# Making the mask and rise tables on the chip, and splitting the first w2 on two engines

## The chip, the cores and the metric

The program runs on one core of a Trainium2 chip. The metric is the time of one execution on the device, in microseconds, lower being better. TensorE (PE in the rows), VectorE (DVE), ScalarE (ACT), GpSimd (POOL) and SyncE (SP) each run their own instruction stream in order and wait for each other through semaphores. DMAs are issued from SyncE's and ScalarE's streams (SPq and ACTq) and are carried by the core's 16 DMA engines.

## The reference

Three stages follow each other. Stage 1 is causal attention with decay (retention): each head has its own gamma, and batch is 2, heads 8, sequence 768, head dimension 64. Stages 2 and 3 are mixtures of experts (8 and 4 experts) over the 1536 x 512 result; stage 2's gates are balanced by eight rounds of row and column normalization.

```python
gamma = 1.0 - 2.0 ** (-5.0 - np.arange(H))
for t in range(S):
    state = gamma[None, :, None, None] * state + einsum('bhd,bhe->bhde', k[:, :, t], v[:, :, t])
    y[:, :, t] = scale * einsum('bhd,bhde->bhe', q[:, :, t], state)
...
for e in range(E):
    h = np.maximum(x @ w1[e], 0.0)
    ye = h @ w2[e]
    out += P[:, e:e + 1] * ye
```

## The kernel before, in words

Stage 1 works in 12 steps, one per chunk of 128 positions and batch (step s is chunk s // 2, batch s % 2). In a step TensorE forms the scores of all 8 heads (`score`, L991), multiplies the raised queries with the running state (L1019, from chunk 1 on), adds this chunk's keys and values to the state in PSUM (L1031, the "kv" part), and multiplies the masked scores with the values (L1037, the "y" part; the last three stand in `attend`, L1004). The scores of step s + 1 are formed before step s is attended to. VectorE multiplies the scores by a table `mask`, which holds gamma to the power of the lag, the scale, and zero above the diagonal (`mask_scores`, L624). GpSimd multiplies the keys by `kdecay` (L349) and the queries by a table `rise` (L362). ScalarE makes the next chunk's `rise` from the one before by a factor `step` (L444).

The tables come from memory. `mask` (512 KB) and `rise` (256 KB) stand in SyncE's queue among the loads of queries, keys and values: the mask behind the keys of step 0, the rise table ahead of step 2. `kdecay`, `step` and the gate weights `wg_raw` are small loads from ScalarE's queue. There are buffers for four steps, so the loads of step 4 wait until step 0 is done (`y_done`), and so on. TensorE first runs 8 matmuls on a zeroed tile (`warm`, L1042), whose results nobody reads, and 3 more after each of the first two `score` calls.

A semaphore wait heads nearly each of these operations; what matters here is that scores need `qk_in` (queries and keys of the step landed) and, from step 2, the masking of two steps before.

From the last steps on, stage 2 begins. Every f32 matrix is split in a high part and a remainder (`x_hi`, `x_lo`; `low`, L666), and a product is three fast matmuls. The first matrix product of an expert's half (`up`, L1094) uses seven sub-products in the manner of Strassen, each in two halves; TensorE's seventh waits for `summed`, which VectorE's `hidden_sum` (L804) raises. `down` (L1134) multiplies with w2, whose parts VectorE makes in `split_w2` (L714). VectorE's own order at this place is written out by hand: the last pieces of x and w1, then all of the first w2 (which has landed in a buffer of its own, `w2_first`), then `hidden(0, 0)`. The rest of the program, about 1480 us, repeats units of `up` and `down`.

Of the kernel before, what the change touches and what calls it, by code (L numbers as in the profile page):

```python
# [14 lines left out]
P = 128  # L15
# [18 lines left out]
WARM, WARM_GAP = 8, 3  # L34
# [27 lines left out]
def retention_moe_moe_kernel(nc, q_t, k_t, k, v, moe_w_gate, moe_w1, moe_w2, moe2_probs, moe2_w1, moe2_w2,  # L62
                             c_ident, c_kdecay, c_mask, c_rise, c_step, out):

    ctx = ExitStack()
    with ctx:
# [15 lines left out]
        with ExitStack() as early:  # L82
            mask = sb("mask", [P, 2, DC, P], F32, early)
            rise = [sb(f"rise{r}", [P, DC, P], F32, early) for r in range(2)]
        w2_hi = sb("w2_hi", [P, UC, DM], F32R)
# [13 lines left out]
        kdecay = sb("kdecay", [P, CH - 1, HEADS])  # L99
        step = sb("step", [P, DC])  # L100
# [36 lines left out]
        ps_kv, ps_y = bank[4], bank[5:8]  # L137
        ps_logit = [bank[6], bank[0]]
# [3 lines left out]
        kdecay_in = sem("kdecay_in")  # L142
        wg_in = sem("wg_in")
        mask_in = sem("mask_in")
        rise_in = sem("rise_in")
# [103 lines left out]
        def _(sp):  # L249
# [93 lines left out]
        def _(pool):  # L343
# [9 lines left out]
            def raise_q(s):  # L353

                c, b = s // BATCH, s % BATCH
                pool.wait_ge(qk_in[c % 2][b], 32 * (c // 2) + 32)
                if c == 1:
                    pool.wait_ge(rise_in, 32)
# [32 lines left out]
            pool.wait_ge(kdecay_in, 16)  # L391
# [24 lines left out]
        def _(act):  # L416
            act.dma_start(kdecay[:, :, :], c_kdecay.rearrange("p (c h) -> p c h", c=CH - 1)).then_inc(kdecay_in, 16)
            act.dma_start(step[:, :], c_step).then_inc(rise_in, 16)
            act.dma_start(wg_raw[:, :, :], moe_w_gate.rearrange("p (c e) -> p c e", e=E1)).then_inc(wg_in, 16)
# [33 lines left out]
            def rise_out(c):  # L453

                if c == 2:
                    act.wait_ge(rise_in, 32)
# [44 lines left out]
            gate_weights()  # L501
            for s in range(STEPS):
# [40 lines left out]
            def unit(k, p, x2=None, first=False):  # L543
# [71 lines left out]
        def _(dve):  # L615
# [98 lines left out]
            def split_w2(k, first=False):  # L714
                raw = w2_first if first else w2_raw
                dve.wait_ge(w2_in, 16 * k + 16)
                if not first:

                    dve.wait_ge(down_done, downs_before(k, 0))
# [12 lines left out]
            dve.wait_ge(mask_in, 16)  # L732
            mask_scores(0)
            dve.wait_ge(wg_hi_ready, 1)
            low(wg_parts[:, :, 64 + E1:64 + 2 * E1], wg_raw[:, :, :], wg_parts[:, :, 64:64 + E1])
            low(wg_parts[:, :, P + E1:P + 2 * E1], wg_raw[:, :, :], wg_parts[:, :, P:P + E1]).then_inc(wg_lo_ready, 1)
            for s in range(STEPS):
# [12 lines left out]
                elif b == 1:  # L750
                    if c < CH - 1:
                        x_low0(c)
                    if c > 0:
                        sums_low(c - 1)
            x_low0(CH - 1)
# [57 lines left out]
            def hidden(k, p, x2=None):  # L813
# [62 lines left out]
            split_w2(0, first=True)  # L876
            hidden(0, 0)
# [100 lines left out]
        def _(pe):  # L978
# [63 lines left out]
            def warm(n):  # L1042

                for i in range(n):
                    nc.tensor.matmul(bank[7][:, 0:P], state[1][:, 0, :], state[1][:, 0, :], start=True, stop=True)
# [165 lines left out]
def _constants():  # L1211
# [6 lines left out]
    lag = pos[None, :] - pos[:, None]  # L1218
    mask = np.where(lag >= 0, gamma[:, None, None] ** np.maximum(lag, 0.0), 0.0) / np.sqrt(HD)
    mask = mask.reshape(DC, 2, P, P).transpose(2, 1, 0, 3)  # L1220
    rise = gamma[:, None] ** (P + 1.0 + pos - SEQ // 2)[None, :] / np.sqrt(HD)
    rise = np.repeat(rise.reshape(DC, 2, 1, P), HD, axis=2).reshape(DC, P, P).transpose(1, 0, 2)
    step = np.repeat((gamma ** float(P)).reshape(DC, 2, 1), HD, axis=2).reshape(DC, P).transpose(1, 0)
    return {
        "c_ident": np.eye(P), "c_kdecay": kdecay.reshape(P, (CH - 1) * HEADS), "c_mask": mask.reshape(P, HEADS * P),
        "c_rise": rise.reshape(P, DC * P), "c_step": step,
# [37 lines left out]
```

## Time and profile before

| | us |
|---|---|
| median of 3 runs | 1552.88 |
| lowest and highest | 1552.87, 1552.95 |
| profiled execution | 1552.96 |
| its span, first to last instruction | 1551.2 |
| TensorE busy | 1543.7 |
| VectorE busy | 880.9 |
| ScalarE busy | 445.2 |
| GpSimd busy | 53.8 |

The span is from the first to the last instruction; the execution's own time has some 1.8 us more around it. TensorE is busy for nearly the whole span, so the reader should look at the few places where it isn't, and at what it is busy with before them: a warming matmul counts as busy too.

### The profile page before, as it was taken

The numbers are of one execution on the slowest core, as the hardware profiler recorded it, in microseconds if no ns is written. First come the engines' busy times: TensorE is split into PE (matmuls) and PEld (weight loads), VectorE is DVE, ScalarE is ACT, GpSimd is POOL, SyncE is SP. The second block draws the span as 40 slices with busy tenths as digits, with TensorE's granted clock in tenths as the row PEclk, the third lists the DMA queues.
The fourth block names the chain that finished last, engine by engine and source line by source line (L and its number), as shares of the span: only waits on it lengthen the run. The fifth ranks groups of instructions, "written<-read, shape, count | busy, mean of one in ns | idle before, by whom it ended". The sixth has DMA issues, their size and how long they took to land.

```text
span 1551.2 us, 21289 instructions
## 1 busy us (share of the span) xinstructions
PE 1543.7 (100%) x8238; PEld 1401.2 (90%) x8238; DVE 880.9 (57%) x1439; ACT 445.2 (29%) x860; POOL 53.8 (3%) x45
## 2 busy tenths in 40 slices
PE   8999999999999999999999999999999999999999
PEld 7989988998899889988998899889998999899988
DVE  6756855546546555465465555567555556555553
ACT  5422331322223213222232132243332223213321
POOL 5300000000000000000000000012000000000000
PEclk9999999999999999999999999999999999999999
DMA  9201101001011010010110100101101001011011
GB/s 341 78 1 55 55 2 55 28 28 55 1 54 54 0 54 27 27 54 2 52 54 0 54 29 26 55 0 55 51 4 55 28 28 55 0 54 54 1 41 68
DMA packets 34891, 67.28 MB, mean 43 GB/s; under 512 B 2320, under 2 KB 2704, under 8 KB 34832
## 3 DMA queue, kind: packets, MB, share of 16 engines
q1 hardware_dynamic: 34400, 66.42, 12.5%
q8 instruction: 41, 0.67, 0.2%
q14 instruction: 18, 0.15, 0.0%
q10 hardware_dynamic: 432, 0.04, 0.0%
HBM read 63.31 MB, written 3.15 MB: 43 GB/s over the span
## 4 chain that ended last, share of the span: by engine, by line
PE 98%; DVE 1%; DMA 0%; SPq 0%; ACT 0%; issue 0%; DVEq 0%
PE bank L1148 17%; PE bank L1149 17%; PE bank L1147 17%; PE bank L1126 15%; PE bank L1130 15%; PE bank L1128 15%; PE bank L999 1%; PE bank L1019 1%; PE bank L1037 1%; PE bank L1031 0%; DVE w_lo L667 0%; DMA qt_in<-in_q_t 0%; PE bank L1090 0%; DVE w_hi L722 0%; DVE x_sum L636 0%; PE bank L1071 0%
## 5 line engine op out<-in xcount | busy, mean ns | idle before, releaser
L1126 PE MATMUL bank<-x_hi,w_hi 128*128 128x384 f32 x1344 | 449.9, 335 | 0.4 <-DVE ups L805 0.4
L1130 PE MATMUL bank<-x_hi,w_lo 128*128 128x384 f32 x1344 | 449.5, 334 | 0.0
L1128 PE MATMUL bank<-x_lo,w_hi 128*128 128x384 f32 x1344 | 449.2, 334 | 0.0
L1149 PE MATMUL bank<-w_hi,h_lo 128*128 128x512 f32 x1148 | 447.6, 390 | 0.0
L1148 PE MATMUL bank<-w_lo,h_hi 128*128 128x512 f32 x1148 | 447.4, 390 | 0.0
L1147 PE MATMUL bank<-w_hi,h_hi 128*128 128x512 f32 x1148 | 446.9, 389 | 0.0
L852 DVE SCALAR_TENSOR_TENSOR acc<-bank,gate,acc 128x512 f32<-128x512 f32 x251 | 188.5, 751 | 372.7 <-PE bank L1149 372.7
L538 ACT COPY ups<-bank 128x384 f32<-128x384 f32 x288 | 138.0, 479 | 902.8 <-PE bank L1130 902.7
L805 DVE TENSOR_TENSOR ups<-bank,ups 128x384 f32<-128x384 f32 x288 | 155.4, 555 | 190.1 <-ACT ups L538 168.4
L1149 PEld LDWEIGHTS bank<-w_hi,h_lo 128*128 128x128 f32 x1148 | 215.4, 188 | 44.9
L1148 PEld LDWEIGHTS bank<-w_lo,h_hi 128*128 128x128 f32 x1148 | 215.4, 188 | 43.8
L1147 PEld LDWEIGHTS bank<-w_hi,h_hi 128*128 128x128 f32 x1148 | 215.5, 188 | 43.6
L1126 PEld LDWEIGHTS bank<-x_hi,w_hi 128*128 128x128 f32 x1344 | 252.3, 188 | 2.9 <-issue 1.1
L1128 PEld LDWEIGHTS bank<-x_lo,w_hi 128*128 128x128 f32 x1344 | 252.3, 188 | 1.8
L1130 PEld LDWEIGHTS bank<-x_hi,w_lo 128*128 128x128 f32 x1344 | 252.2, 188 | 0.0
L541 ACT ACTIVATE h_hi<-ups 128x384 fp32r<-128x384 f32 x288 | 148.3, 526 | 135.7 <-DVE ups L805 135.7
L810 DVE SCALAR_TENSOR_TENSOR h_lo<-ups,h_hi 128x384 fp32r<-128x384 f32 x288 | 156.3, 557 | 12.3
L667 DVE TENSOR_TENSOR w_lo<-w_raw,w_hi 128x1024 fp32r<-128x1024 f32 (+1 forms) x95 | 112.7, 1207 | 0.0
L810 DVE SCALAR_TENSOR_TENSOR h_lo<-bank,h_hi 128x384 fp32r<-128x384 f32 x96 | 53.5, 558 | 2.2
L541 ACT ACTIVATE h_hi<-bank 128x384 fp32r<-128x384 f32 x96 | 47.3, 493 | 12.5
L367 POOL TENSOR_TENSOR x_lo<-x_sum,x_hi 128x1024 fp32r<-128x1024 f32 x7 | 17.9, 2559 | 894.3 <-ACT x_hi L442 894.3
L667 DVE TENSOR_TENSOR w_lo<-w_sum,w_hi 128x1024 fp32r<-128x1024 f32 (+1 forms) x48 | 46.4, 966 | 0.0
(96 smaller groups left out, 508.4 us busy)
## 6 DMA issues: line engine op xcount, KB each, us to landing
w_raw<-in_moe_w SPq DMA_DIRECT2D x46, 1024.0 KB, 5.0
kt_in<-in_k_t SPq DMA_DIRECT2D x12, 256.0 KB, 3.9
qt_in<-in_q_t SPq DMA_DIRECT2D x12, 256.0 KB, 5.2
v_in<-in_v SPq DMA_DIRECT2D x12, 256.0 KB, 5.6
k_in<-in_k SPq DMA_DIRECT2D x10, 256.0 KB, 5.4
out<-acc SPq DMA_DIRECT2D x2, 768.0 KB, 3.5
out<-acc SPq DMA_DIRECT2D x5, 256.0 KB, 2.0
w_raw<-in_moe_w SPq DMA_DIRECT2D x4, 256.0 KB, 5.6
```

Of the source, the lines that this page charges most:

```text
L538: nc.scalar.copy(ups[:, half, slot, :], up_psum(ON_X, half)).then_inc(copied, 1)
L541: nc.scalar.activation(h_hi[:, f, b, :], src, ACT.Relu).then_inc(h_hi_ready, 1)
L667: return nc.vector.tensor_tensor(out, raw, high.bitcast(F32), ALU.subtract)
L805: nc.vector.tensor_tensor(ups[:, half, slot, :], up_psum(kind, half), ups[:, half, slot, :], ALU.add).then_inc(summed, 1)
L810: nc.vector.scalar_tensor_tensor(h_lo[:, f, b, :], src, 0.0, h_hi[:, f, b, :].bitcast(F32), ALU.max, ALU.subtract).then_inc(h_ready, 1)
L852: nc.vector.scalar_tensor_tensor(a, y, gate[:, i, bass.ds(col, 1)], a, ALU.mult, ALU.add).then_inc(acc_written, 1)
L1126: nc.tensor.matmul(o, w1_hi[:, w, kc, fs], x_hi[:, x, kc, at], start=start and kc == 0, stop=False, skip_group_check=True)
L1128: nc.tensor.matmul(o, w1_hi[:, w, kc, fs], x_lo[:, x, kc, at], start=False, stop=False, skip_group_check=True)
L1130: last = nc.tensor.matmul(o, w1_lo[:, w, kc, fs], x_hi[:, x, kc, at], start=False, stop=kc == 1, skip_group_check=True)
L1147: nc.tensor.matmul(o, h_hi[:, f, b, rows], w2_hi[:, f, :], start=(n == 0), stop=False)
L1148: nc.tensor.matmul(o, h_hi[:, f, b, rows], w2_lo[:, f, :], start=False, stop=False)
L1149: last = nc.tensor.matmul(o, h_lo[:, f, b, rows], w2_hi[:, f, :], start=False, stop=(n == UC - 1))
```

## The change

The tables are no longer loaded. A new constant `rows` has one row for each head (8 rows of 1792 numbers, 56 KB): gamma to the power of minus the key's position, a row that marks the head's parity, gamma to the power of the query's position with the scale (each head in its own block of 128 columns), and the rise. A matmul of `rows` with itself over 8 partitions gives gamma to the power of query minus key for four heads at once, 512 columns wide: two such matmuls make the mask (one for each parity of the head), a third the rise. VectorE multiplies the first two by a table `causal` (64 KB, zero above the diagonal) into `mask`, and ScalarE copies the third into `rise`. `kdecay` and `step` come in one load, `small`. The gate weights load from SyncE's queue after step 3, and their splitting goes into step 5 on ScalarE and step 6 on VectorE. Of the warming matmuls 3 of the 14 stay. The high parts of the first w2 are copied by ScalarE in its first unit, and VectorE makes the remainders between two parts of `hidden(0, 0)`.

```diff
-WARM, WARM_GAP = 8, 3
+WARM = 3
...
-            sp.dma_start(mask[:, :, :, :], c_mask.rearrange("p (r c j) -> p r c j", r=2, c=DC)).then_inc(mask_in, 16)
...
-                if s == 2:
-                    sp.dma_start(rise[1][:, :, :], c_rise.rearrange("p (c t) -> p c t", c=DC)).then_inc(rise_in, 16)
...
+                if s == 3:
+                    sp.dma_start(wg_raw[:, :, :], moe_w_gate.rearrange("p (c e) -> p c e", e=E1)).then_inc(wg_in, 16)
...
             def _(act):
-            act.dma_start(kdecay[:, :, :], c_kdecay.rearrange("p (c h) -> p c h", c=CH - 1)).then_inc(kdecay_in, 16)
-            act.dma_start(step[:, :], c_step).then_inc(rise_in, 16)
-            act.dma_start(wg_raw[:, :, :], moe_w_gate.rearrange("p (c e) -> p c e", e=E1)).then_inc(wg_in, 16)
+            act.dma_start(rows[:, :], c_rows).then_inc(rows_in, 16)
+            act.dma_start(small[:, :], c_small).then_inc(small_in, 16)
+            act.dma_start(causal[:, :], c_causal).then_inc(causal_in, 16)
...
-            gate_weights()
+            act.wait_ge(tables_done, 3)
+            nc.scalar.copy(rise[1][:, :, :], ps_rise[:, :].rearrange("p (c t) -> p c t", c=DC)).then_inc(rise_made, 1)
...
+                if s == 5:
+                    gate_weights()
...
                     hidden_copy(k, p, 3, half, U_U4)
+                if first:
+                    act.wait_ge(w2_in, 16)
+                    for g in range(2):
+                        at = slice(2 * g, 2 * g + 2)
+                        nc.scalar.copy(w2_hi[:, at, :], w2_first[:, at, :]).then_inc(w2_hi_ready, 1)
...
+            def first_w2_low():
+                for g in range(2):
+                    at = slice(2 * g, 2 * g + 2)
+                    dve.wait_ge(w2_hi_ready, g + 1)
+                    low(w2_lo[:, at, :], w2_first[:, at, :], w2_hi[:, at, :]).then_inc(w2_ready, 1)
...
-            dve.wait_ge(mask_in, 16)
+            dve.wait_ge(causal_in, 16)
+            for r in range(2):
+                dve.wait_ge(tables_done, r + 1)
+                nc.vector.tensor_tensor(mask[:, r, :, :], ps_mask[r][:, :].rearrange("p (c i) -> p c i", c=DC),
+                                        causal[:, :].unsqueeze(1).to_broadcast([P, DC, P]),
+                                        ALU.mult).then_inc(mask_made, 1)
+            dve.wait_ge(mask_made, 2)
             mask_scores(0)
...
                     hidden_sum(k, p, half, half, U_U4, ON_Y)
+                if first:
+                    first_w2_low()
...
             pe.wait_ge(zeroed, 4)
             warm(WARM)
+            pe.wait_ge(rows_in, 16)
+            for r in range(2):
+                nc.tensor.matmul(ps_mask[r][:, :], row_keys, row_query[r], start=True, stop=True).then_inc(tables_done, 1)
             score(0)
-            warm(WARM_GAP)
+            nc.tensor.matmul(ps_rise[:, :], row_parity, row_rise, start=True, stop=True).then_inc(tables_done, 1)
+            pe.wait_ge(mask_made, 2)
             for s in range(STEPS):
                 if s < STEPS - 1:
                     score(s + 1)
-                if s == 0:
-                    warm(WARM_GAP)
                 attend(s)
```

The first place is TensorE's stream at the very start (`state` is the zeroed tile of the warming matmuls, `qt_in,kt_in` are scores, `v_in,k_dec` the kv part, `scores,v_in` the y part). Before:

```order
L1045 MATMUL bank<-state 128x128 [waits zeroed]
L1045 MATMUL bank<-state 128x128 x7
L999 MATMUL bank<-qt_in,kt_in 128x128 [waits qk_in00]
L999 MATMUL bank<-qt_in,kt_in 128x128 x7
L1045 MATMUL bank<-state 128x128 x3
L999 MATMUL bank<-qt_in,kt_in 128x128 [waits qk_in01]
L999 MATMUL bank<-qt_in,kt_in 128x128 x7
L1045 MATMUL bank<-state 128x128 x3
L1031 MATMUL bank<-v_in,k_dec 64x64 [waits k_decayed,v_in_s00]
L1031 MATMUL bank<-v_in,k_dec 64x64 x7
L1037 MATMUL bank<-scores,v_in 64x128 [waits masked]
```

Now (the line numbers are those of the changed file):

```order
L1080 MATMUL bank<-state 128x128 [waits zeroed]
L1080 MATMUL bank<-state 128x128 x2
L1086 MATMUL bank<-rows 128x512 [waits rows_in]
L1086 MATMUL bank<-rows 128x512
L1034 MATMUL bank<-qt_in,kt_in 128x128 [waits qk_in00]
L1034 MATMUL bank<-qt_in,kt_in 128x128 x7
L1088 MATMUL bank<-rows 128x512
L1034 MATMUL bank<-qt_in,kt_in 128x128 [waits qk_in01,mask_made]
L1034 MATMUL bank<-qt_in,kt_in 128x128 x7
L1066 MATMUL bank<-v_in,k_dec 64x64 [waits k_decayed,v_in_s00]
L1066 MATMUL bank<-v_in,k_dec 64x64 x7
```

Five of the eight first warming matmuls are gone, two of 512 columns stand in front of the first scores and one behind them instead of three warming ones; the three warming ones between the second scores and the kv part have gone with nothing in their place, and the second scores wait for `mask_made`.

The second place is VectorE's stream at the first w2 (the casts are the high parts, `w_lo<-w_first` the remainders, `ups<-bank,ups` is `hidden_sum`). Before:

```order
L722 CAST w_hi<-w_first 128x1024 [waits w2_in]
L722 CAST w_hi<-w_first 128x1024
L667 TENSOR_TENSOR w_lo<-w_first,w_hi 128x1024 [waits w2_hi_ready] x2
L805 TENSOR_TENSOR ups<-bank,ups 128x384 [waits copied] x2
L810 SCALAR_TENSOR_TENSOR h_lo<-ups,h_hi 128x384 [waits h_hi_ready]
L810 SCALAR_TENSOR_TENSOR h_lo<-bank,h_hi 128x384 [waits h_hi_ready]
L810 SCALAR_TENSOR_TENSOR h_lo<-ups,h_hi 128x384 [waits h_hi_ready]
L810 SCALAR_TENSOR_TENSOR h_lo<-bank,h_hi 128x384 [waits h_hi_ready]
L805 TENSOR_TENSOR ups<-bank,ups 128x384 [waits up_done] x2
```

Now:

```order
L689 TENSOR_TENSOR w_lo<-w_sum,w_hi 128x512 [waits w1_hi_ready]
L689 TENSOR_TENSOR w_lo<-w_raw,w_hi 128x2x2x256 [waits w1_hi_ready]
L839 TENSOR_TENSOR ups<-bank,ups 128x384 [waits copied] x2
L689 TENSOR_TENSOR w_lo<-w_first,w_hi 128x1024 [waits w2_hi_ready] x2
L844 SCALAR_TENSOR_TENSOR h_lo<-ups,h_hi 128x384 [waits h_hi_ready]
L844 SCALAR_TENSOR_TENSOR h_lo<-bank,h_hi 128x384 [waits h_hi_ready]
L844 SCALAR_TENSOR_TENSOR h_lo<-ups,h_hi 128x384 [waits h_hi_ready]
L844 SCALAR_TENSOR_TENSOR h_lo<-bank,h_hi 128x384 [waits h_hi_ready]
L839 TENSOR_TENSOR ups<-bank,ups 128x384 [waits up_done] x2
L844 SCALAR_TENSOR_TENSOR h_lo<-ups,h_hi 128x384 [waits h_hi_ready] x2
```

The two casts have left this engine, and the two remainders stand behind the first two `hidden_sum` instead of ahead of them.

The third is ScalarE's stream at the same place (`ups<-bank` are the copies of sub-products, `h_hi` the high parts of the hidden layer). Before:

```order
L538 COPY ups<-bank 128x384 [waits up_done] x2
L442 CAST x_hi<-x_sum 128x8x128 [waits x_summed]
L538 COPY ups<-bank 128x384 [waits up_done] x2
L541 ACTIVATE h_hi<-ups 128x384 [waits summed]
L541 ACTIVATE h_hi<-bank 128x384 [waits up_done]
L541 ACTIVATE h_hi<-ups 128x384 [waits summed]
```

Now:

```order
L555 COPY ups<-bank 128x384 [waits up_done] x2
L455 CAST x_hi<-x_sum 128x8x128 [waits x_summed]
L555 COPY ups<-bank 128x384 [waits up_done] x2
L577 CAST w_hi<-w_first 128x1024 [waits w2_in]
L577 CAST w_hi<-w_first 128x1024
L558 ACTIVATE h_hi<-ups 128x384 [waits summed]
L558 ACTIVATE h_hi<-bank 128x384 [waits up_done]
L558 ACTIVATE h_hi<-ups 128x384 [waits summed]
```

The two casts now stand here, between the last copies and the first `h_hi`.

## Rows read from the trace of the kernel before

**Rows 1.** What TensorE waited for, whole run: total us, times, longest

```profile
PE bank L1045 <- DVE bank L731: 2.6, 1, 2.6
PE bank L999 <- DMA qt_in<-in_q_t: 1.7, 1, 1.7
PE bank L1126 <- DVE ups L805: 0.4, 1, 0.4
```

**Rows 2.** Timeline: ScalarE's first and third load, TensorE's start: start, duration

```profile
0.73 0.41 ACTq L417 DMA_DIRECT2D kdecay<-in_c_kdecay  x1
1.65 0.45 ACTq L419 DMA_DIRECT2D wg_raw<-in_moe_w_gate  x1
2.62 3.46 PE L1045 MATMUL bank<-state 128*128 128x128 f32 x16 [2.62 <-DVE bank L731]
6.01 1.16 PE L999 MATMUL bank<-qt_in,kt_in 64*128 64x128 f32 x16
```

**Rows 3.** Chain that ended last, first 17 us: start, duration, what

```profile
3.53 6.12 DMA qt_in<-in_q_t
9.69 1.16 PE bank L999 x16
10.85 0.86 PE bank L1045 x6
11.72 0.62 PE bank L1031 x16
12.33 0.88 PE bank L1037 x16
13.21 1.09 PE bank L999 x16
...
15.79 1.16 PE bank L999 x16
```

**Rows 4.** DMA issues, first 70 us: count, KB, us to landing

```profile
mask<-in_c_mask SPq DMA_DIRECT2D x1, 512.0 KB, 5.5
kdecay<-in_c_kdecay ACTq DMA_DIRECT2D x1, 20.0 KB, 3.1
wg_raw<-in_moe_w_gate ACTq DMA_DIRECT2D x1, 16.0 KB, 4.2
```

**Rows 5.** Windows view, 10 to 16 us: engines' busy time, clock, DMA share, GB/s

```profile
10.00:16.00 6.00, 6.00 (x104) 5.22 (x102) 2.89 (x5) 3.42 (x10) 3.50 (x4) 1.00 1.06 393
```

**Rows 6.** Timeline of GpSimd, the two waits for queries of chunk 1

```profile
13.10 1.27 POOL L362 TENSOR_TENSOR q_up<-qt_in,rise 128x512 f32<-128x512 f32 x1 [1.65 <-DMA qt_in<-in_q_t]
15.81 1.27 POOL L362 TENSOR_TENSOR q_up<-qt_in,rise 128x512 f32<-128x512 f32 x1 [0.44 <-DMA qt_in<-in_q_t]
```

**Rows 7.** Query load of step 4: issued, us to landing, and its first user

```profile
13.62 0.43 SPq L253 DMA_DIRECT2D qt_in<-in_q_t  x1
qt_in<-in_q_t SPq DMA_DIRECT2D x1, 256.0 KB, 5.4
19.46 1.16 PE L999 MATMUL bank<-qt_in,kt_in 64*128 64x128 f32 x16
```

**Rows 8.** Timeline of VectorE: first masking, and a steady step

```profile
7.66 1.29 DVE L630 TENSOR_TENSOR scores<-bank,mask 128x512 f32<-128x512 f32 x2 [5.09 <-DMA mask<-in_c_mask]
28.06 1.29 DVE L630 TENSOR_TENSOR scores<-bank,mask 128x512 f32<-128x512 f32 x2 [0.67 <-PE bank L999]
```

**Rows 9.** Timeline of VectorE and ScalarE round the first w2

```profile
57.43 3.50 DVE L722 CAST w_hi<-w_first 128x1024 fp32r<-128x1024 f32 x2
63.12 1.01 DVE L805 TENSOR_TENSOR ups<-bank,ups 128x384 f32<-128x384 f32 x2
53.90 1.05 ACT L490 CAST w_hi<-w_raw 128x1024 fp32r<-128x1024 f32 x1
59.25 0.48 ACT L538 COPY ups<-bank 128x384 f32<-128x384 f32 x1 [0.56 <-PE bank L1130]
```

**Rows 10.** Chain again: the first matmul of the first down

```profile
71.68 0.23 PE bank L1147
```

More of the change, by code:

```diff
@@ L84, in retention_moe_moe_kernel @@
             rise = [sb(f"rise{r}", [P, DC, P], F32, early) for r in range(2)]
+            rows = sb("rows", [HEADS, 2 * P + 3 * DC * P], F32, early)
+            causal = sb("causal", [P, P], F32, early)
+            row_keys, row_parity = rows[:, 0:P], rows[:, P:2 * P]
+            row_query = [rows[:, 2 * P + r * DC * P:2 * P + (r + 1) * DC * P] for r in range(2)]
+            row_rise = rows[:, 2 * P + 2 * DC * P:2 * P + 3 * DC * P]
         w2_hi = sb("w2_hi", [P, UC, DM], F32R)
@@ L98, in retention_moe_moe_kernel @@
         neg_gmax = sb("neg_gmax", [P, 1])
-        kdecay = sb("kdecay", [P, CH - 1, HEADS])
-        step = sb("step", [P, DC])
+        small = sb("small", [P, (CH - 1) * HEADS + DC])
+        kdecay = small[:, 0:(CH - 1) * HEADS].rearrange("p (c h) -> p c h", c=CH - 1)
+        step = small[:, (CH - 1) * HEADS:(CH - 1) * HEADS + DC]
         sb("place", [P, 128])
@@ L141, in retention_moe_moe_kernel @@
         ident_in = sem("ident_in")
-        kdecay_in = sem("kdecay_in")
+        small_in = sem("small_in")
+        rows_in = sem("rows_in")
+        causal_in = sem("causal_in")
+        tables_done = sem("tables_done")
+        mask_made = sem("mask_made")
+        rise_made = sem("rise_made")
         wg_in = sem("wg_in")
-        mask_in = sem("mask_in")
-        rise_in = sem("rise_in")
         wg_zeroed = sem("wg_zeroed")
@@ L712, in split_w1_low, with split_w2 @@
                         w1_hi[:, at, :, :].rearrange("p m k f -> p k m f")).then_inc(w1_ready, 1)
[L714 to L715 removed]
+            def first_w2_low():
[3 more added lines that the diff above has]
+                    low(w2_lo[:, at, :], w2_first[:, at, :], w2_hi[:, at, :]).then_inc(w2_ready, 1)
+            def split_w2(k):
+                raw = w2_raw
                 dve.wait_ge(w2_in, 16 * k + 16)
[L717 to L719 removed]
+                dve.wait_ge(down_done, downs_before(k, 0))
                 for g in range(2):
@@ L754, in _ @@
                         sums_low(c - 1)
+                if s == 6:
+                    dve.wait_ge(wg_hi_ready, 1)
+                    low(wg_parts[:, :, 64 + E1:64 + 2 * E1], wg_raw[:, :, :], wg_parts[:, :, 64:64 + E1])
+                    low(wg_parts[:, :, P + E1:P + 2 * E1], wg_raw[:, :, :], wg_parts[:, :, P:P + E1]).then_inc(wg_lo_ready, 1)
             x_low0(CH - 1)
@@ L811, in hidden_low, with hidden @@
                                                ALU.max, ALU.subtract).then_inc(h_ready, 1)
-            def hidden(k, p, x2=None):
+            def hidden(k, p, x2=None, first=False):
                 if x2 is not None:
@@ L874, in unit @@
                 down(k, 1, gate, col, how, split_next=True)
-            split_w2(0, first=True)
-            hidden(0, 0)
+            hidden(0, 0, first=True)
             down(0, 0, gate1, 0, "copy")
@@ L1044, in warm @@
                 for i in range(n):
-                    nc.tensor.matmul(bank[7][:, 0:P], state[1][:, 0, :], state[1][:, 0, :], start=True, stop=True)
+                    nc.tensor.matmul(bank[6][:, 0:P], state[1][:, 0, :], state[1][:, 0, :], start=True, stop=True)
             pe.wait_ge(zeroed, 4)
             warm(WARM)
+            pe.wait_ge(rows_in, 16)
+            for r in range(2):
+                nc.tensor.matmul(ps_mask[r][:, :], row_keys, row_query[r], start=True, stop=True).then_inc(tables_done, 1)
             score(0)
-            warm(WARM_GAP)
+            nc.tensor.matmul(ps_rise[:, :], row_parity, row_rise, start=True, stop=True).then_inc(tables_done, 1)
+            pe.wait_ge(mask_made, 2)
             for s in range(STEPS):
@@ L1217, in _constants @@
     kdecay = (gamma[None, :] ** keys[:, None]).reshape(CH - 1, P, HEADS).transpose(1, 0, 2)
-    lag = pos[None, :] - pos[:, None]
-    mask = np.where(lag >= 0, gamma[:, None, None] ** np.maximum(lag, 0.0), 0.0) / np.sqrt(HD)
-    mask = mask.reshape(DC, 2, P, P).transpose(2, 1, 0, 3)
+    step = np.repeat((gamma ** float(P)).reshape(DC, 2, 1), HD, axis=2).reshape(DC, P).transpose(1, 0)
+    parity = (np.arange(HEADS)[:, None] % 2 == np.arange(P)[None, :] // HD).astype(np.float64)
+    query = gamma[:, None] ** pos[None, :] / np.sqrt(HD)
     rise = gamma[:, None] ** (P + 1.0 + pos - SEQ // 2)[None, :] / np.sqrt(HD)
-    rise = np.repeat(rise.reshape(DC, 2, 1, P), HD, axis=2).reshape(DC, P, P).transpose(1, 0, 2)
-    step = np.repeat((gamma ** float(P)).reshape(DC, 2, 1), HD, axis=2).reshape(DC, P).transpose(1, 0)
+    blocks = np.zeros((HEADS, 3, DC, P))
+    for h in range(HEADS):
+        blocks[h, h % 2, h // 2] = query[h]
+        blocks[h, 2, h // 2] = rise[h]
+    rows = np.concatenate([gamma[:, None] ** -pos[None, :], parity, blocks.reshape(HEADS, 3 * DC * P)], axis=1)
     return {
-        "c_ident": np.eye(P), "c_kdecay": kdecay.reshape(P, (CH - 1) * HEADS), "c_mask": mask.reshape(P, HEADS * P),
-        "c_rise": rise.reshape(P, DC * P), "c_step": step,
+        "c_ident": np.eye(P), "c_small": np.concatenate([kdecay.reshape(P, (CH - 1) * HEADS), step], axis=1),
+        "c_rows": rows, "c_causal": pos[None, :] >= pos[:, None],
     }
```

13 lines of the change are left out of this document (6 added, 7 removed).

## The prediction

> **What bounds the kernel now.** I read the whole-run waits of TensorE first, since it is busy for nearly the whole span. In all 1551.2 us it waits three times: 2.6 us for the first memsets, 1.7 us for the queries of step 1, and 0.4 us for VectorE's `hidden_sum` [rows 1]. Nothing after the first `up` makes it wait. So a change can only gain in the first 72 us: by one of these waits, or by work on TensorE itself. It cannot touch the 2.6 us.
>
> Then the timeline and the chain of the first 16 us. TensorE starts at 2.62, runs eight warming matmuls until 6.01 (0.424 us each) and then the first scores [rows 2]. The chain comes through the load of the queries of step 1, which TensorE takes up at 9.69. From there it is TensorE alone: scores 1.1, three warming matmuls 0.86 (0.287 each), kv 0.62, y 0.88, scores of step 2 1.09, kv and y again 1.5, and the scores of step 3 at 15.79 [rows 3]. The reader is to see two things: the 0.86 are filler on the chain, and the same 128-column matmul costs 0.424 before 6.01 and 0.287 later. The granted clock reads 1.00 (2.4 GHz) for 10 to 16 us [rows 5]; for the slower stretch before 6.01 I go by the durations, and call it the slow rate.
>
> The third view is of who waits for the loads. GpSimd waits for the queries of step 2 until 13.10 and of step 3 until 15.81, where TensorE's scores start at 13.2 and 15.79 [rows 3, 6]. So for the steps 1, 2 and 3 TensorE runs exactly as the loads land, and the filler alone is worth nothing without faster loads. The DMA engines are fully used, at 393 GB/s [rows 5]. From step 4 on there is a margin: its queries land at 13.62 + 5.4 = 19.0, its scores start at 19.46 [rows 7], and the loads are spaced closer than the 3.67 us of a step (19.46 - 15.79).
>
> **The loads.** Out of SyncE's queue go the mask (512 KB [rows 4]), which stands ahead of the queries of step 1, and the rise (256 KB), ahead of those of step 2. In come 56 KB of rows, 64 KB of causal and 22 KB of small constants, against 38 KB that leave ScalarE's queue: 0.105 MB more. At 393 GB/s the mask is 0.524 / 393 = 1.33 us, both tables 2.00 us, and the new bytes 0.27 us. The queries should land: step 1 by 9.69 - 1.33 + 0.27 = 8.6, step 2 at 13.10 - 1.73 = 11.4, step 3 at 15.81 - 1.73 = 14.1, step 4 at 19.0 - 1.7 = 17.3. The issue of step 4's loads waits for `y_done` of step 0, which comes earlier too (below). The 16 KB of gate weights that now pass ahead of it are 0.04 us.
>
> How the 56 KB are spread matters. The Trainium skill (DMA: Bandwidth & Descriptors, "Why a DMA increments its semaphore by 16 and not by 1") says that a load over 8 rows can use only 8 of the 16 engines. The trace has no such load. By the rule those 8 engines carry 7 KB each at 393 / 16 = 24.6 GB/s, 0.29 us instead of 0.15, and the queries of step 3 would land at 14.2, and the sum would be 0.15 smaller. The sum goes without it.
>
> **TensorE's start.** Three warming matmuls end at 2.62 + 3 x 0.424 = 3.89. The rows are the first load of ScalarE's queue. Their nearest row is the load that stood there: issued at 0.73, landed 3.1 later, at 3.83 [rows 2, 4]. The ends are nothing lost (3.89) and the mask's own 5.5 (6.2). I take 3.89, as the load is small and first.
>
> A 512-column f32 matmul does not occur in the trace. At the later rate, four 128-column ones are 4 x 0.287 = 1.15, and four passes at the 0.23 of a 512-column matmul of `down` 0.92 [rows 3, 10]; I take 1.0. At the rate before 6.01 it is 4 x 0.424 = 1.70. That the rate changes at 6.01 again I take from this trace. Then: first mask matmul 3.89 to 5.59; the second has done 0.42 / 1.70 = a quarter by 6.01 and ends at 6.77; scores of step 0 (1.09) 7.86; rise 8.86. The scores of step 1 can start then, since their queries are there at 8.6. They also wait for `mask_made`: VectorE's two multiplications are like its maskings, 1.29 for two [rows 8]; `causal` is the third load, 1.65 + 4.2 = 5.85 by the row of its place, at worst 1.65 + 5.5 = 7.2 [rows 2, 4]. The second ends at 6.77 + 0.65 = 7.4 or, at the worst, 8.5, before 8.86. Behind it on VectorE wait only the maskings of step 0, which end at 9.3 or 9.8; y of step 0 needs them at 10.6.
>
> From 8.86: scores 1.09, kv 0.62, y 0.88 give 11.45 (queries of step 2 are there at 11.4), 1.09 + 0.62 + 0.88 more give 14.04, and the queries of step 3 land at 14.1. So these scores start at 14.1 instead of 15.79: 1.7 us gained, and both the loads and the filler had to give way for it. ScalarE's copy of the rise (about 0.6, over half of the 1.05 of a twice as wide cast [rows 9]) is done at 9.5, and GpSimd needs it at 11.4. Behind that copy ScalarE has the state copies of step 0, wanted at 10.6. Step 4 would need its queries at 14.1 + 3.67 = 17.8 and has them at 17.3.
>
> The margin of step 3 is nil, so both ends follow: with rows at 3.83 and 0.92 a matmul TensorE comes out 0.2 earlier, but the loads hold it at 14.1 (13.8 if the new bytes ran beside the others for nothing). With the dear matmul (1.15) it is 0.4 later, 14.5. That is a gain of 1.3 to 2.0.
>
> **The gate weights.** Two small copies on ScalarE and two on VectorE (0.28 us) move into steps 5 and 6. VectorE has 0.67 us idle ahead of a masking in such a step [rows 8], and TensorE wants the weights only after the first `up`. I cost them at nothing; without this cover they would cost 0.3.
>
> **The first w2.** VectorE starts its two casts at 57.43, takes 3.50 for them and comes to `hidden_sum` only at 63.12, so TensorE waits 0.4 us [rows 1, 9]. Now `hidden_sum` needs ScalarE's second copy, done at 59.73 [rows 9], so both are done 3 us before TensorE asks. The whole 0.44 goes. What is late next? ScalarE's two casts of 1024 columns cost 1.05 each [rows 9]: 59.73 to 61.8. The remainders on VectorE follow, to about 63.1, where VectorE used to start `hidden_sum`; it is now 1.0 ahead with these two done. The first `down` starts at 71.68 [rows 10] and asked for no wait before, so this hides. I value it at 0.44, with ends 0 and 0.5.
>
> **Sum.** Against the profiled execution of 1552.96: 1.7 + 0.44 = 2.1, so 1550.8. The median of the runs is 0.08 below that execution, which changes nothing beyond 0.1; I say 1550.8.
>
> **Rivals.** (a) *The rate rises late.* The warming stretch is shorter and may have a hole before the rows. In this trace the fast rate comes after 3.39 us of uninterrupted matmuls. If it came only at 9.4 (a point assumed for the price), the two mask matmuls end at 7.29, scores (1.09 x 0.424 / 0.287 = 1.61) at 8.90, rise at 10.1, and the scores of step 3 start at 15.3: 0.5 + 0.44 gained, 1552.0. For it: TensorE's first 3.4 us now hang on a load. Against: if the rows land at 3.83 there is no hole, and the two mask matmuls keep it busy. The Trainium skill (TensorE: Matmul & The Clock Gate, "Part 1: The HAM clock gate") says that the throttled state is the default, that sustained activity releases it, and that the point of release differs from run to run of one kernel. The trace agrees with the first, 0.424 against 0.287 us; a shift of the point is what this rival prices, and by the rule it has a chance in any run.
>
> (b) *Slower: the rate stays low through the whole start.* With 3 warming matmuls, a hole, and later waits for loads, it stays at 0.424. Slow until the end of step 1's scores gives 3.89 + 3.40 + 1.61 + 1.70 + 1.61 = 12.2, and with the 4.09 that follow (0.62 + 0.88 + 1.09 + 0.62 + 0.88) at the fast rate the scores of step 3 stand at 16.3; with the 0.44 of the w2 this is break-even. So it decides at 12.2. Slow to the end of that stretch (5.10 for the three wide matmuls, and 1.09 + 1.09 + 4.09 = 6.27 times 0.424 / 0.287) gives 3.89 + 14.4 = 18.2, 2.4 later than 15.79, net 2.0 slower: 1555.0. Against it: TensorE idled 1.7 us before 9.69 [rows 1] and the three matmuls behind ran fast.
>
> (c) *The rows come late.* If they land as the mask did, at 6.2, and TensorE is at its fast rate, its 3.0 + 6.27 = 9.3 us of work end at 15.5: 0.3 + 0.44 gained, 1552.2.
>
> (d) *The loads do not land sooner.* The traffic of steps 2 and 3 moves up less than the bytes say, and step 3 starts at 15.8 as before. Only the 0.44 is left: 1552.5. Against: 1.00 and more of DMA share throughout [rows 5].
>
> (e) *More gain.* The loads of the start get better than their bytes, since many tiny pieces leave ScalarE's queue, and the rate rises early: step 3 at 13.3, 1550.0.
>
> **How the numbers follow.** The forecast has 0.62, (a) 0.13, (b) 0.05, (c) 0.07, (d) 0.06, (e) 0.07. The forecast's own range is 1550.4 to 1551.3; taking in (a), (c) and (e) it is 1549.9 to 1552.3, which leaves out (b) and (d). About what a measurement of this kernel can tell from no change is 0.2%, here 3.1 us. All the cases but the tails of (e) and (b) lie within it: faster by more 0.06, slower by more 0.02, the same 0.92.
>
> **What would show it.** TensorE's timeline: 3 warming matmuls to 3.9, mask matmuls of 1.7 and about 1.2, scores of step 1 at 8.9, of step 3 at 14.1. The waits of TensorE: no row for the first `hidden_sum`, none for `rows`, at most some tenths for queries and for VectorE's mask. The first `down` at 71.68 - 2.1 = 69.5. The prediction is wrong if the mask matmuls are slow both, if step 3's scores stand later than 14.6 or before 13.7, or if a wait in the first `up` or `down` comes up.

## The result and the profile after

The changed kernel takes 1556.36 us (median of 13 runs, 1554.92 to 1557.53), the kernel before 1552.95 (13 runs, 1552.46 to 1553.37). The ratio is 1.0022, with a 95% interval of 1.0013 to 1.0030: 3.4 us slower, where 2.1 us faster was forecast. The profiled execution took 1556.92, its span 1555.1, TensorE's busy time 1549.0. The spread is part of the result: 2.6 us against 0.9.

The waits of TensorE over the whole run, where before had the three of [rows 1]:

```profile
PE bank L1080 <- DVE bank L758: 2.6, 1, 2.6
PE bank L1054 <- DVE x_sum L658: 0.8, 1, 0.8
```

Both waits that the change was to remove are gone: none for the queries of step 1 (which TensorE now asks for only at 11.98), none for `hidden_sum`. One of 0.8 us for x_sum has come. But the loss does not stand among the waits. It is in the chain (start, duration, what), which answers to [rows 2, 3, 10]:

```profile
2.61 1.65 PE bank L1080 x6
4.27 3.71 PE bank L1086 x4
7.97 2.01 PE bank L1034 x16
9.98 2.00 PE bank L1088 x2
11.98 2.01 PE bank L1034 x16
13.99 1.05 PE bank L1066 x16
15.04 1.71 PE bank L1072 x16
16.75 1.34 PE bank L1034 x16
...
19.58 1.09 PE bank L1034 x16
...
75.64 0.23 PE bank L1185
```

The reader should compare durations. The scores of steps 0 and 1 take 2.01 where they took 1.1 [rows 3], kv 1.05 for 0.62, y 1.71 for 0.88. Two mask matmuls take 3.71, the rise 2.00. Only inside the scores of step 2 (1.34, between 2.01 and 1.09) does TensorE get fast, near 17 us; before, it was fast at 6.01 [rows 2]. So the scores of step 3 start at 19.58 instead of 15.79, 3.8 later. The first `down` starts at 75.64 instead of 71.68, 4.0 later, as much as the two profiled executions differ (1556.92 - 1552.96): 3.8 of slow rate, 0.8 of the new wait, less 0.4 for the w2, with 0.2 of small differences left.

The loads did what was forecast: the queries of step 3 are issued at 7.34 and land 6.3 us later, at 13.6, where 14.1 was forecast. In the windows view (stretch, then busy time of PE, PEld, DVE, ACT, POOL, clock, DMA share, GB/s) they are all in by 14, and the DMA engines idle, since the loads of step 4 wait for TensorE (their queries are issued at 17.16 instead of 13.62 [rows 7]):

```profile
14.00:16.00 2.00, 2.00 (x28) 2.00 (x30) 1.29 (x2) 0.88 (x3) 0.82 (x2) 1.00 0.07 17
```

The granted clock reads 1.00 from the start of this trace on, although the durations until near 17 are about twice the fast ones. In no trace of this case does that column show the slow start; in the first 20 us it reads 0.50 only in two runs below, where the clock fell after it had been up. For the start the durations have to be compared.

### The profile page after: what moved, and what is told of

The parts are those of the page before. It is cut to its first block, busy times and chain, and to the rows that moved or that the text cites. A ratio compares the mean times of both kernels' runs of the same rounds, so it can differ in the third digit from the quotient of the medians.

```text
span 1555.1 us, 21262 instructions
## 1 busy us (share of the span) xinstructions
PE 1549.0 (100%) x8222; PEld 1402.5 (90%) x8222; DVE 881.7 (57%) x1439; ACT 447.7 (29%) x863; POOL 54.3 (3%) x45
## 4 chain that ended last, share of the span: by engine, by line
PE 98%; DVE 1%; ACT 0%; issue 0%; DVEq 0%
PE bank L1186 17%; PE bank L1187 17%; PE bank L1185 17%; PE bank L1164 15%; PE bank L1168 15%; PE bank L1166 15%; PE bank L1034 1%; DVE x_lo L689 0%; PE bank L1072 0%; PE bank L1128 0%; PE bank L1054 0%; DVE scores L652 0%; DVE x_sum L658 0%; PE bank L1086 0%; PE bank L1066 0%
## 5 line engine op out<-in xcount | busy, mean ns | idle before, releaser
L844 DVE SCALAR_TENSOR_TENSOR h_lo<-ups,h_hi 128x384 fp32r<-128x384 f32 x288 | 156.1, 557 | 12.2
```

The lines of the kernel that those rows point to most:

```text
L844: nc.vector.scalar_tensor_tensor(h_lo[:, f, b, :], src, 0.0, h_hi[:, f, b, :].bitcast(F32), ALU.max, ALU.subtract).then_inc(h_ready, 1)
```

## The experiments

**The w2 part alone**, on the kernel before (its `first_w2_low` and the two casts in ScalarE's first unit):

```diff
-            split_w2(0, first=True)
-            hidden(0, 0)
+            hidden(0, 0, first=True)
```

> The kernel before with only the w2 part of the change: the first high parts of w2 on ScalarE, the remainders behind the first two hidden_sum on VectorE. Theory (the w2 part gives what it was priced at): the 0.4 us wait of TensorE for hidden_sum goes, about 0.4 us faster than before, 1552.5. Rival (the w2 part costs something that the changed kernel hides): no gain or slower, with a new wait in the first up or down.

Measured: 1552.45 (11 runs) against 1552.99 for before, measured beside it, ratio 0.9996 (0.9987 to 1.0004). The waits:

```profile
PE bank L1056 <- DVE bank L741: 2.6, 1, 2.6
PE bank L1010 <- DMA qt_in<-in_q_t: 1.2, 1, 1.2
```

The wait for `hidden_sum` is gone and none has come. The gain of 0.5 fits the 0.44 of the forecast, though the interval cannot tell it from none.

**8 warming matmuls in the changed kernel:**

```diff
-WARM = 3
+WARM = 8
```

> The changed kernel with 8 first warming matmuls instead of 3. Theory A (TensorE stays at its slow rate since too little full work stood in front of the loads' rows): the fast rate is there at 6.0, the mask matmuls start at 6.0 and take some 1.0 each instead of 1.9, the scores of step 3 start at about 15.3 instead of 19.5; about 1552.8, that is 3.6 us faster than the changed kernel. Rival B (the slow rate comes from the wide 8-row matmuls themselves, whatever stands ahead): they and the scores behind them stay slow (2.0), the scores of step 3 start at 21 or later, and the time is 1 to 2 us above the changed kernel's.

Measured: 1557.17 (1552.60 to 1558.80, 12 runs), no better than with 3, and the widest spread of all: two of the runs lie at 1552.6, where theory A put them, and the other ten at 1555.9 and more. The profiled one (1556.18) is one of the ten. The timeline of TensorE (start, duration, line, count):

```profile
6.33 2.04 PE L1086 MATMUL bank<-rows 8*128 8x512 f32 x4
8.30 1.16 PE L1034 MATMUL bank<-qt_in,kt_in 64*128 64x128 f32 x16
9.39 1.60 PE L1088 MATMUL bank<-rows 8*128 8x512 f32 x2
10.92 2.08 PE L1034 MATMUL bank<-qt_in,kt_in 64*128 64x128 f32 x16
```

and the windows:

```profile
9.00:10.00 1.00, 1.00 (x12) 0.56 (x8) 0.54 (x2) 0.00 (x0) 0.79 (x1) 0.95 1.05 406
10.00:12.00 2.00, 2.00 (x12) 1.08 (x12) 0.85 (x2) 0.59 (x1) 0.24 (x1) 0.50 1.05 399
...
14.00:16.00 2.00, 2.00 (x20) 1.67 (x18) 0.32 (x1) 1.87 (x6) 1.79 (x2) 0.50 0.05 14
16.00:17.00 1.00, 1.00 (x14) 1.00 (x14) 0.00 (x0) 0.73 (x2) 0.47 (x1) 0.64 0.28 53
17.00:20.00 3.00, 3.00 (x55) 2.59 (x54) 2.27 (x4) 1.38 (x4) 1.04 (x1) 1.00 0.92 306
```

Theory A holds until 9: the warming matmuls bring the fast rate, the mask matmuls take 2.04 together and the first scores 1.16. Then the clock falls to 0.50 (1.2 GHz) inside the rise matmul, without any pause of TensorE, and stays there until after 16. What TensorE had done since 6.33 were two 8-row matmuls, one set of scores and part of the third 8-row matmul. So neither theory was right as it stood: in this execution full warming brought the clock up, and it fell during the table matmuls. (The last run of this section has the same 8 warming matmuls ahead of table matmuls over 128 rows, and no fall.)

**The gate weights back at the start of the changed kernel** (load from ScalarE's queue, copies ahead of the rise copy, subtractions behind the first masking):

```diff
-                if s == 5:
-                    gate_weights()
...
+            gate_weights()
             act.wait_ge(tables_done, 3)
```

> The changed kernel with the gate weights' load and splitting put back to the start. Theory (the two small VectorE subtractions, which took 1.99 us together where they stand now, made VectorE late and so TensorE wait 0.8 us near 52): that wait goes, 0.8 us faster than the changed kernel, about 1555.6. Rival (VectorE is late anyway because TensorE's stream no longer leaves it idle time, or because of collisions with GpSimd): the wait stays at 0.5 or more, within 0.3 us of the changed kernel.

Measured: 1555.93 (11 runs), 1.0018 of before (1.0009 to 1.0026). No wait of TensorE is left in the trace but the first, of 2.6. The two subtractions take 0.28 again. The scores of step 3 start at 18.82, so 0.76 of the 1.60 that this execution (1555.32) is below the changed kernel's profiled one belongs to the clock, which rose earlier. The other 0.84 fit the wait; the medians differ by 0.43 only.

**The kernel before with its warming matmuls on 8 partitions:**

```diff
-nc.tensor.matmul(bank[7][:, 0:P], state[1][:, 0, :], state[1][:, 0, :], start=True, stop=True)
+nc.tensor.matmul(bank[7][:, 0:P], state[1][0:8, 0, :], state[1][0:8, 0, :], start=True, stop=True)
```

> The kernel before with all its 14 warming matmuls over 8 partitions instead of 128; same columns, same count. Theory A1 (matmuls over 8 rows do not bring the fast rate): the first scores take 2.0 instead of 1.1, the fast rate comes some microseconds later, the scores of step 3 start at 17 to 19 instead of 15.8, and the time is 1.5 to 3.5 us above before. Rival A2 (rows do not matter, only the time that TensorE has been busy): the fast rate at 6.0 as before, 1552.9, no change.

Measured: 1556.75 (11 runs), ratio 1.0024 (1.0016 to 1.0033). Nothing but the number of rows has changed, and the whole loss is there:

```profile
2.61 3.78 PE L1045 MATMUL bank<-state 8*128 8x128 f32 x16 [2.61 <-DVE bank L731]
6.32 2.08 PE L999 MATMUL bank<-qt_in,kt_in 64*128 64x128 f32 x16
8.33 1.64 PE L1045 MATMUL bank<-state 8*128 8x128 f32 x6
10.05 2.08 PE L999 MATMUL bank<-qt_in,kt_in 64*128 64x128 f32 x16
...
16.39 1.44 PE L999 MATMUL bank<-qt_in,kt_in 64*128 64x128 f32 x16
```

The 14 matmuls have the same columns and last as long as full ones at the slow rate (3.78 for 8 here, 3.79 for the 8 full ones of the changed kernel with 8 warming matmuls). The scores take 2.08 at 6.32 and at 10.05, and the rate changes at 16.39 or later. A1 is shown, A2 falls. The loss of 3.8 and step 3 at 19.25 lie a little beyond what A1 had expected (at most 3.5, and 19).

**Half the rows, 64,** with the same edit:

> The kernel before with all its 14 warming matmuls over 64 partitions instead of 128. If half the rows are enough, the fast rate is there at about 6 as before and the time is 1552.9. If only full rows bring it, the first scores are slow (2.0) and the time is like that of the 8-row warming, about 1556.7.

Measured: 1552.89, but 7 of the 11 runs lie between 1552.55 and 1553.19 and 4 between 1554.55 and 1555.73. In the profiled one (1552.74) the first scores still take 1.96 and those of step 1, at 9.39, 1.16. Half the rows bring the clock up, later, and not early enough in every run. Neither expectation holds alone.

**3 first warming matmuls in the kernel before:**

```diff
-WARM, WARM_GAP = 8, 3
+WARM, WARM_GAP = 3, 3
```

> The kernel before with 3 first warming matmuls instead of 8 (the later ones and all loads as before). Theory A (full-row work is missing, whoever takes it away): TensorE idles from 3.9 until the first queries, the fast rate is not there at 6.0, scores of step 0 take about 2.0, and the scores of step 3 start at 17 or later: 1 to 4 us above before. Rival (3 warming matmuls are enough, and only the 8-row matmuls hold the rate down): fast rate as before, within 0.3 us of before.

Measured: 1554.51 (1552.84 to 1556.14) against 1553.08 for before, ratio 1.0010 (1.0001 to 1.0019). The timeline and the windows:

```profile
4.32 1.92 PE L999 MATMUL bank<-qt_in,kt_in 64*128 64x128 f32 x16
9.53 2.08 PE L999 MATMUL bank<-qt_in,kt_in 64*128 64x128 f32 x16 [2.43 <-DMA qt_in<-in_q_t]
```

```profile
8.00:10.00 2.00, 0.47 (x4) 0.47 (x6) 1.01 (x4) 0.00 (x0) 0.00 (x0) 0.84 1.05 400
10.00:12.00 2.00, 2.00 (x18) 1.78 (x17) 0.36 (x1) 0.00 (x0) 1.04 (x1) 0.50 1.05 402
12.00:14.00 2.00, 2.00 (x32) 1.88 (x33) 0.93 (x2) 0.30 (x1) 1.07 (x1) 0.81 1.06 387
```

The clock was up near 6 (the three warming matmuls at 6.16 take 0.94 together, against 1.65 for the first three), but TensorE then had 2.4 us to wait for the queries of step 1, and the clock went to 0.50 there (0.84 over 8 to 10) and came back between 12 and 14. So fewer warming matmuls cost 1.4 us by themselves in the median, less than the 8-row ones do. The expectation of slow scores of step 0 was right (1.92), and so was that of step 3 at 17 or later (17.04). Its reason was right only in part: TensorE did not idle before the first scores, and the later loss came from the fall during the wait.

**Full rows: the changed kernel with `rows` filled to 128 partitions by zeros,** gate weights at the start, 3 warming matmuls:

```diff
-            act.dma_start(rows[:, :], c_rows).then_inc(rows_in, 16)
+            act.dma_start(rows[0:32, :], c_rows).then_inc(rows_in, 16)
...
+            nc.gpsimd.memset(rows[64:128, :], 0.0).then_inc(rows_zeroed, 1)
...
+            nc.vector.memset(rows[32:64, :], 0.0).then_inc(rows_zeroed2, 1)
```

> The changed kernel with the gate weights back at the start, and with the rows tile filled to 128 partitions by zeros (32 rows loaded, the rest set by memset), so that the three wide matmuls run over all 128 rows; only 3 warming matmuls. Theory A (rows decide): they count as full work, the fast rate is there between 5.6 and 7, the scores of step 3 start at 14.3 to 15.0, about 1551.3, below before by 1.2 to 2. Rival C (wide matmuls with few weight loads do not bring the fast rate, whatever their rows): slow until about 16 as in the run with the gate weights at the start, 1555.5 to 1556.

Measured: 1551.79 (11 runs) against 1553.08 for before, ratio 0.9993 (0.9984 to 1.0002); the same kernel once more 1552.26 against 1553.35. Its chain:

```profile
4.68 2.89 PE bank L1090 x4
7.57 1.09 PE bank L1036 x16
8.66 1.05 PE bank L1092 x2
9.71 1.09 PE bank L1036 x16
...
14.88 1.09 PE bank L1036 x16
```

Two mask matmuls now take 2.89, the second at the fast rate, and all behind them is fast: scores 1.09, rise 1.05. The scores of step 3 start at 14.88. TensorE waits 0.4 us for the memset, its only wait behind the first. This execution (1551.32) is the fastest of its 11. In the profiled one of the repeat (1552.89) both mask matmuls are slow (3.78), the rate changes only inside the first scores (1.54, past 9), and step 3 starts at 16.36. So full rows bring the rate up in every trace of this kernel and its variants with 3 warming matmuls, but at a point between about 6.5 and 9.5.

Against the gate-weights run, the same but for the rows (24 of the 120 rows of zeros are loaded, 224 KB instead of 56, and 96 are set by memset), the medians are 4.1 us apart. Rival C falls.

**The loads put back** into the full-rows kernel, 512 and 256 KB at their old places, into a buffer free at that time:

```diff
+            sp.dma_start(w2_raw[:, 0:2, :], moe_w2[0, 0:2 * P, :].rearrange("(c p) n -> p c n", p=P)).then_inc(extra_in, 16)
...
+                if s == 2:
+                    sp.dma_start(w2_raw[:, 2, :], moe_w2[0, 2 * P:3 * P, :]).then_inc(extra_in, 16)
```

> The full-rows kernel with loads of 512 and 256 KB put back at the places of the mask and the rise in SyncE's queue, into a buffer that nobody reads then. If the loads bound steps 2 and 3, the scores of step 3 go from 14.8 back to 15.8 to 16.2, and the time is 0.8 to 1.3 us above the full-rows run. If only the TensorE's rate mattered, they stay at 14.8 and the time at 1551.8.

Measured: 1553.22 (11 runs, 1552.94 to 1553.55), 1.4 above the full-rows run:

```profile
10.38 1.16 PE L1042 MATMUL bank<-qt_in,kt_in 64*128 64x128 f32 x16 [0.20 <-DMA qt_in<-in_q_t]
13.69 1.16 PE L1042 MATMUL bank<-qt_in,kt_in 64*128 64x128 f32 x16 [0.65 <-DMA qt_in<-in_q_t]
16.40 1.16 PE L1042 MATMUL bank<-qt_in,kt_in 64*128 64x128 f32 x16
```

TensorE waits for the queries of steps 1 and 2, and step 3 stands at 16.40, 1.5 later than in the chain of the full-rows run and 0.2 beyond the expected end of 16.2. Fewer loads are worth about what was worked out (1.7), once TensorE is fast.

**No filler, tables loaded** (the w2 run without the second `warm(WARM_GAP)`):

```diff
-                if s == 0:
-                    warm(WARM_GAP)
```

> The kernel before with the w2 part of the change and without the three warming matmuls between the scores of step 1 and the kv part (0.86 us on the chain); tables still loaded. The prediction's claim (TensorE waits for the loads of steps 2 and 3 anyway): the scores of step 3 still start at 15.8, within 0.2 us of the w2 run (1552.45). Rival (the loads have a margin): 0.5 to 0.9 us faster than that run.

Measured: 1552.31 against 1552.45 of the w2 run. The wait of 0.73 ahead of the scores of step 2, which the w2 run does not have, is the filler's 0.86 come back as waiting (the wait of 1.83 ahead of step 1 stands before the filler's place):

```profile
9.92 1.16 PE L1010 MATMUL bank<-qt_in,kt_in 64*128 64x128 f32 x16 [1.83 <-DMA qt_in<-in_q_t]
13.31 1.16 PE L1010 MATMUL bank<-qt_in,kt_in 64*128 64x128 f32 x16 [0.73 <-DMA qt_in<-in_q_t]
16.02 1.16 PE L1010 MATMUL bank<-qt_in,kt_in 64*128 64x128 f32 x16
```

**The gate weights late in the full-rows kernel:**

> The full-rows kernel with the gate weights' load and splitting at steps 3, 5 and 6, as in the changed kernel. Theory (VectorE's two small subtractions collide with GpSimd there and take 1.99 us instead of 0.28, VectorE stays late): TensorE waits 0.5 to 1 us for x_sum near 48 to 50, and the time is 0.5 to 1 us above the full-rows run (1551.8). The prediction's value: nothing, within 0.2 us of it.

Measured: 1552.78, 1.0 above, but its profiled execution (1552.28) had no such wait; its clock rose later instead (3.70 for the two mask matmuls). Its two subtractions took 1.08 together and the `x_lo` subtractions behind them their usual 1.22. So this left the question open. **The move alone, on the kernel before:**

```diff
+                if s == 6:
+                    dve.wait_ge(wg_hi_ready, 1)
+                    low(wg_parts[:, :, 64 + E1:64 + 2 * E1], wg_raw[:, :, :], wg_parts[:, :, 64:64 + E1])
```

> The kernel before with only the gate weights moved: their load behind step 3 in SyncE's queue, ScalarE's copies in step 5, VectorE's subtractions in step 6. Theory D (the move costs by itself): VectorE is late from step 6 on, TensorE waits for x_sum or masks near 48, 0.5 to 1 us above before. Rival E (the move costs only where the slow start has shifted VectorE and GpSimd against each other): within 0.2 us of before, no new wait of TensorE.

Measured: 1553.98 against 1553.35 for before, ratio 1.0002 (0.9993 to 1.0011). The 11 runs fall in two groups: 4 at 1552.95 to 1553.18, 7 at 1553.81 to 1554.33. The profiled one is of the second (waits, and two pieces of the chain):

```profile
PE bank L1022 <- DVE x_sum L638: 0.8, 1, 0.8
PE bank L1129 <- DVE ups L808: 0.4, 1, 0.4
```

```profile
34.74 0.54 DVE wg_parts L669
35.56 1.08 DVE wg_parts L669
```

The wait of 0.8 for x_sum is the same as in the changed kernel, with the clock undisturbed, so E, which wanted a slow start for it, falls. That the seven of the upper group are those with the wait is likely, but only one was profiled; and the interval over all 11 does not exclude zero.

The full-rows pair once more, side by side:

> The full-rows kernel once more, beside the next one on the same chip. Both theories: 1551.8 within 0.3, with the fast rate beginning between 5.5 and 9.

> The full-rows kernel with the gate weights late, once more beside it. Theory D: 0.5 to 1.2 us above it again, also where the fast rate begins at the same time, with a wait of TensorE for VectorE in its trace. Rival E: the 1.0 of the first time was chance in when the fast rate began, and the two agree within 0.3.

Measured: 1552.26 and 1552.70, 0.4 apart, with spreads of 1.6 and 2.9. The trace of the late one again had no wait for x_sum (its subtractions took 0.18 and 0.99), only the 0.4 for the memset. The early one's fast rate began past 9, later than expected. This pair tells D from E no better than the first.

**Two variations of the full-rows kernel:** the memset in two pieces, and with it 8 warming matmuls.

```diff
-            nc.vector.memset(rows[32:64, :], 0.0).then_inc(rows_zeroed2, 1)
+            nc.vector.memset(rows[32:64, 0:2 * P + 2 * DC * P], 0.0).then_inc(rows_zeroed2, 1)
+            nc.vector.memset(rows[32:64, 2 * P + 2 * DC * P:], 0.0).then_inc(rows_zeroed2, 1)
```

> The full-rows kernel with VectorE's memset of the zero rows in two pieces, the one that the mask matmuls need first, so that they need not wait 0.4 us for it. Expected 0.2 to 0.4 us faster than the full-rows run, 1551.5; a version meant to beat both kernels. If the loads of steps 2 and 3 bind at once, nothing is gained.

> The same with 8 warming matmuls. The mask matmuls start at 6.1 and run at the fast rate; scores of step 3 at about 15.2, some 0.5 us later than with 3, about 1552.0. If the warming matmuls of the changed kernel were too few in themselves, this is the faster one instead.

Measured: 1552.15 (1551.10 to 1553.54) and 1552.54 (1552.09 to 1553.19), before 1553.07. Neither expectation came true. In the first the wait for the memset became one of 0.2 for the rows, but in its profiled execution both mask matmuls were slow (3.78) and step 3 stood at 15.92: the point where the rate rises weighs more than the wait, and its median is not below the full-rows run's. The second is 0.8 above the full-rows run, with the steadier time: its mask matmuls started at 6.19 and took 2.61, not all of it at the fast rate, and step 3 stood at 16.04 instead of 15.2. From there on every set of scores takes 1.16 in the timeline. Behind the same 8 warming matmuls, the clock fell with 8-row table matmuls, with times spread over 6.2 us, and stayed up with 128-row ones, with a spread of 1.1 (this kernel also has its gate weights early). Full rows with 3 warming matmuls stays the version with the lowest medians (1551.79 and 1552.26), 1.1 to 1.3 us below before each time, and over 4 below the changed kernel's 1556.36. Its slowest execution (1553.22) is faster than the changed kernel's fastest (1554.92), so that it beats the changed kernel is shown. The interval of its ratio to before still reaches 1.0002 each time, so that it beats before is likely and not shown.

## Why the prediction was wrong

**The failed step** is the one under TensorE's start that says "That the rate changes at 6.01 again I take from this trace". It took the time of the change from a stretch of 8 full-row matmuls and used it for 3 of these followed by matmuls over 8 rows. I had compared work by how long TensorE was occupied. The run with 8-row warming shows that occupation is not enough: the same columns and the same time on 8 partitions leave the rate slow, and cost 3.8 us. The full-rows run shows the rest: with 128 rows behind the same 3 warming matmuls, 4.1 us come back. Even there 6.01 does not hold: the rate rises between about 6.5 and 9.5. In the terms of the sum, step 3 was to start at 14.1 and started at 19.58: the gain of 1.7 became a loss of 3.8. Of the three signs of being wrong that the prediction names, the first two came up (both mask matmuls slow, step 3 later than 14.6).

**Rival (b)** had the right effect, at a chance of 0.05. It put break-even at a rise at 12.2 and priced a wholly slow stretch with step 3 at 18.2; it rose near 17 and step 3 stood at 19.58, since the slow scores cost 2.01 and not the 1.61 that the warming matmuls' ratio gave. That ratio was read wrongly: the 0.424 before 6.01 is not all slow. The first 8 matmuls take 3.46 in before and 3.78 where the rate stays slow, so in before it had risen inside them, near 5.7. Its cause was misjudged, a hole in the work; there was no hole. Its counter-argument, that the three matmuls behind a wait of 1.7 us ran fast, holds for full warming; behind 3 first warming matmuls and a wait of 2.4 us the clock did fall.

**The Trainium skill's rule** on the clock (TensorE: Matmul & The Clock Gate, "Part 1: The HAM clock gate": throttled by default, released by sustained activity) was read as speaking of time alone. The traces agree with it: the rate is slow at first (0.47 us a warming matmul in the 8-row run, 3.78 for 8) and fast behind full-row work. But I took the busy column for the activity, and the 8-row run shows the two apart. How the chip weighs rows no run here shows, only that 8, 64 and 128 of them differ.

**The size of the wide matmul** was right at the fast rate: 1.0 taken, 1.05 measured in the full-rows run. At the slow rate it was 1.70 against 1.86 (3.71 for two).

**The loads** were right: all in by 14, and the loads-back run loses 1.4. While TensorE was slow they seem to have been worth nothing: the 8-row warming run, with all tables loaded, takes 1556.75 and waits for no load either. The filler is worth nothing alone, as was said.

**The rows' landing** was taken at 3.89, and the mask matmuls started at 4.27 right behind the warming ones (0.55 each here, not 0.424), with no wait for the rows: that fits, and shows no more than a landing by 4.27.

**The w2:** 0.44 forecast, no wait left in the trace, 0.5 between medians, within the noise.

**The gate weights** are the second term that failed: they were costed at nothing, on the 0.67 us of idle VectorE time, and 0.8 us stand in the changed kernel's trace. In their new place the two subtractions take up to 1.99 us instead of 0.28, beside GpSimd's `k_dec` and `q_up`:

```profile
38.46 1.99 DVE L689 TENSOR_TENSOR wg_parts<-wg_raw,wg_parts 128x32 fp32r<-128x32 f32 x2
39.35 1.05 POOL L362 TENSOR_TENSOR k_dec<-k_in,small 128x512 f32<-128x512 f32 x1
...
42.17 1.98 DVE L689 TENSOR_TENSOR x_lo<-x_sum,x_hi 128x1024 fp32r<-128x1024 f32 x1
43.02 2.03 POOL L362 TENSOR_TENSOR k_dec<-k_in,small 128x512 f32<-128x512 f32 x1
```

The cover was sized for the duration they had in an empty place. In the changed kernel's trace this and a subtraction of 1.98 (1.22 elsewhere) make VectorE late and TensorE wait 0.8. The traces divide: in the three with subtractions of 1.98 or 1.99 (this one, the one with 8 warming matmuls, the move on the kernel before) TensorE waits 0.8 for x_sum, and in the two with 1.08 and 1.09 (late gate weights on full rows) it doesn't. In the chain of this one the second subtraction starts at 39.37 and ends at 40.45, and `k_dec` runs from 39.35 to 40.40 in the rows above: it looks as if the one waited for the other. What the two engines collide on was not tried; that they overlap in the rows is what is shown.

## What to carry to other kernels

When matmuls stand in for warming ones, compare how many partitions they cover and not only how long they keep TensorE busy: here 8 partitions did not do what 128 did, and 120 rows of zeros brought most of the loss back. A time read from a trace (the change at 6.01) belongs to the work that stood before it, and varies between executions. And a small operation moved into an idle gap must be priced at the duration it will have beside its new neighbours.

## What the runs showed of the hardware

- 14 warming matmuls on 8 partitions left TensorE at the slow rate until after 16, on 64 partitions until between 8 and 9 in the profiled execution, and on 128 until about 6 to 7 (scores already fast at 6.0 in three traces, the change inside the matmuls that start at 6.19 and 6.33 in two others).
- The clock fell to 0.50 in a stretch where TensorE never paused, during 8-row matmuls (8 warming matmuls in the changed kernel, 9 to 10 us), and also in a wait of 2.4 us after a short start.
- Behind the same 8 full warming matmuls, table matmuls on 128 partitions kept the clock up in the profiled execution.
- Where the start depends on this, single executions of one kernel differ by up to 6.2 us (1552.60 to 1558.80), against 1.5 for the kernel before, measured beside it (1552.34 to 1553.87).
- Two VectorE subtractions of 32 columns took 0.28 us in an empty place, and 1.08 to 1.99 beside GpSimd's work.
